# The last gated slice in two halves of tokens, and the last block's outputs in four stores

## The chip, the cores and the metric

One core of one Trainium2 chip runs the whole program. The metric is device time in microseconds (us), the median of the runs shown. TensorE is called PE here (its weight loads PEld), VectorE DVE, ScalarE ACT, GpSimd POOL, SyncE SP. SP issues the transfers that matter in this case.

## The reference, cut to what matters

A recurrence over the sequence gives 3072 tokens of width 384, a layer of experts changes some of them, and a gated layer ends the program:

```
a = x @ w1                       # x 3072 x 384, w1 384 x 1024
b = x @ w2
h = a * b @ w3                   # w3 1024 x 1024
return h @ w_out                 # w_out 1024 x 384
```

Only that last layer is touched. The kernel has already multiplied w3 by w_out into one matrix wf (1024 x 384), so what is left is g = (x w1) * (x w2) and out = g wf. Each fp32 operand is split into a high and a low part, and each product is made of three matmuls: high by high, high by low, low by high.

## The kernel before, in words

The function `gated_layers` works through 3072 tokens in NB = 6 blocks of TOK = 512. A block has KF = 8 slices of 128 gates. Gates of one slice (`gates(t, f)`, L1515) are 2 weights x 3 chunks of the width x 3 parts = 18 matmuls with 512 moving columns, the tokens of the block; they fill two banks of PSUM, `p_ab[f % 2][0]` for a and `[1]` for b. The outputs of one slice (`outputs(t, f)`, L1527) are 4 token blocks x 3 parts = 12 matmuls with 384 moving columns. They have g of the slice as weights and add up over the 8 slices in four banks `p_o[0..3]`, one for each block of 128 tokens.

Between gates and outputs of a slice stands a chain of four operations on 128x512: ACT copies a out of PSUM (L1574), DVE multiplies it by b (L1612), ACT rounds the product to its high part g_hi (L1577), DVE takes the low part g_lo (L1614). To cover it, PE makes the gates of slice f before the outputs of slice f-1 (`step`, L1544): gates 0, outputs 7 of the block before, gates 1, outputs 0, ..., gates 7, outputs 6, and so on. After the gates 7 of the last block there are only outputs 6 left and then outputs 7. a_sb, g_sb, g_hi, g_lo exist twice, by f % 2.

When a block's outputs are done, ACT copies `p_o[0]` and `p_o[2]` and DVE `p_o[1]` and `p_o[3]` to `o_sb` (L1588, L1632). The helper `first_or_all` lets the copies of blocks 0 and 1 start once `s_o` says that `p_o[1]` is complete, and those of 2 and 3 once `s_gout` says that all four are. SP then stores two halves of 256 tokens each (L1485 to L1490), each after one ACT copy and one DVE copy, and waits at the end for all stores (L1493). The order on each engine is written out by hand; the six blocks run as two unrolled, a loop over the middle, two unrolled and one more step that holds only outputs 7 of the last block.

Of the kernel before, what the change touches and what calls it, by code (L numbers as in the profile page):

```python
# [9 lines left out]
ALU = mybir.AluOpType  # L10
ACT = mybir.ActivationFunctionType
AX = mybir.AxisListType
P = 128


def wait(eng, s, val):

    if isinstance(val, int) and val <= 0:
        return
    eng.wait_ge(s, val)  # L20
# [977 lines left out]
class ExpertInputs:  # L998
# [32 lines left out]
    def part(self, g):  # L1031
        return slice(2 * g * P, 2 * (g + 1) * P)
# [390 lines left out]
def gated_layers(nc, env, xbuf, out):  # L1423

    N, DM = xbuf.shape
    TOK = 4 * P
    NB = N // TOK
    NI = TOK // P
    wm_hi, wm_lo, ident, fold = (env[k] for k in ("wm_hi", "wm_lo", "ident", "fold"))
    KD, KF = DM // P, fold.KF  # L1430
    with ExitStack() as ctx:
# [24 lines left out]
        wf_hi, wf_lo = sb("wf_hi", [P, KF, DM], F32R), sb("wf_lo", [P, KF, DM], F32R)  # L1456
        s_wfhi, s_wflo = sem("wfhi"), sem("wflo")

        def first_or_all(eng, t, i):

            if i < NI // 2:
                wait(eng, s_o, t.num(1, 1))
            else:
                wait(eng, s_gout, t.num(KF, KF))
# [8 lines left out]
        with nc.Block() as block:  # L1473
            @block.sync
            def _(sp):
                def load(t):
                    if isinstance(t.c, int) and t.num() == 0:
                        return
                    if isinstance(t.c, int) and t.num() == 2:
                        sp.wait_ge(s_T, 2)  # L1480
                    else:
                        wait(sp, s_turned, t.num(KD, -2 * KD))
                    gx.load(sp, xbuf, t.slot, t.num())

                def store(t):  # L1485
                    for h in range(2):
                        wait(sp, s_oact, t.num(2, h + 1))
                        wait(sp, s_odve, t.num(2, h + 1))
                        sp.dma_start(out[bass.ds(t.num(TOK, h * TOK // 2), TOK // 2), :].rearrange("(i p) d -> p i d", p=P),
                                     o_sb[t.slot][:, 2 * h:2 * h + 2, :]).then_inc(s_st[t.slot], 16)  # L1490
                rounds(sp, whole((load, 2), (store, 0)), 2, NB, 2, 0)
                for i in range(2):
                    sp.wait_ge(s_st[i], 32 * NB // 2)  # L1493

            @block.gpsimd
            def _(pool):
# [4 lines left out]
            @block.tensor  # L1501
            def _(pe):
                fold.product(pe, KF - 1, p_o[-1], (2,))
                pe.wait_ge(env["s_wmlo"], 2 * KD)

                def first_transposes(part):

                    for i in range(NI):
                        if part == 0 and i % 2 == 0:
                            pe.wait_ge(s_x[i // 2], 16)  # L1510
                        for k in ((0, 1), (2,))[part]:
                            m = pe.transpose(p_ab[part][k % 2][:, i * P:(i + 1) * P], x_in[0][:, i, k * P:(k + 1) * P], ident[:, :])
                    m.then_inc(s_T, 1)

                def gates(t, f):  # L1515
                    wait(pe, s_g, t.num(KF, f - 1))
                    cols = slice(f * P, (f + 1) * P)
                    for w in range(2):
                        for k in range(KD):
                            if f == 0 and w == 0:  # L1520
                                wait(pe, s_xlo, t.num(KD, k + 1))
                            for n, (a, b) in enumerate(((wm_hi, xT_hi), (wm_hi, xT_lo), (wm_lo, xT_hi))):
                                m = pe.matmul(p_ab[f % 2][w][:, :], a[:, w * KD + k, cols], b[t.slot][:, k, :],  # L1523
                                              start=(k == 0 and n == 0), stop=(k == KD - 1 and n == 2))
                    m.then_inc(s_ab, 1)

                def outputs(t, f):  # L1527
                    wait(pe, s_glo, t.num(KF, f + 1))
                    if isinstance(t.num(), int) and t.num() == 0:
                        pe.wait_ge(s_wflo, f + 1)  # L1530
                        pe.wait_ge(fold.s_Wout, KF)
                    if f == 0:
                        wait(pe, s_oact, t.num(2))
                        wait(pe, s_odve, t.num(2))
                    for i in range(NI):
                        cols = slice(i * P, (i + 1) * P)
                        for n, (a, b) in enumerate(((g_hi, wf_hi), (g_hi, wf_lo), (g_lo, wf_hi))):
                            m = pe.matmul(p_o[i][:, 0:DM], a[f % 2][:, cols], b[:, f, :],  # L1538
                                          start=(f == 0 and n == 0), stop=(f == KF - 1 and n == 2))
                        if f == KF - 1 and i == NI // 2 - 1:  # L1540
                            m.then_inc(s_o, 1)
                    m.then_inc(s_gout, 1)

                def step(c, j):  # L1544
                    t, before = Item(c, j, 0, 2), Item(c, j, -1, 2)
                    for f in range(KF):
                        if t.inside(NB):
                            gates(t, f)
                        if f:
                            if t.inside(NB):  # L1550
                                outputs(t, f - 1)
                        elif before.inside(NB):
                            outputs(before, KF - 1)
                first_transposes(0)
                first_transposes(1)
                fold.product(pe, KF - 1, p_o[-1], (3,))
                rounds(pe, step, 2, NB, 0, 1)

            @block.scalar
            def _(act):  # L1560
                def wf_part(f):
                    act.wait_ge(fold.s_Wout, f + 1)
                    act.activation(wf_hi[:, f, :], fold.wf[:, f, :], ACT.Copy).then_inc(s_wfhi, 1)

                def wf_parts():

                    for f in range(KF):
                        if f == KF - 1:
                            fold.taken(act, f, p_o[-1])
                        wf_part(f)  # L1570

                def product(t, f):
                    wait(act, s_ab, t.num(KF, f + 1))
                    act.activation(a_sb[f % 2][:, :], p_ab[f % 2][0][:, :], ACT.Copy).then_inc(s_a, 1)  # L1574
                    wait(act, s_g, t.num(KF, f + 1))
                    wait(act, s_gout, t.num(KF, f - 1))
                    act.activation(g_hi[f % 2][:, :], g_sb[f % 2][:, :], ACT.Copy).then_inc(s_ghi, 1)  # L1577

                def first_x_hi():
                    for k in range(KD):  # L1580
                        act.wait_ge(s_T, 1 + k // 2)
                        act.activation(xT_hi[0][:, k, :], p_ab[k // 2][k % 2][:, :], ACT.Copy).then_inc(s_xhi, 1)

                def x_hi(t, k):
                    wait(act, s_turned, t.num(KD, k + 1 - KD))
                    act.activation(xT_hi[t.slot][:, k, :], xT[:, k, :], ACT.Copy).then_inc(s_xhi, 1)

                def out_copy(t):  # L1588
                    wait(act, s_st[t.slot], t.turn(32))
                    for i in range(0, NI, 2):  # L1590
                        first_or_all(act, t, i)
                        act.activation(o_sb[t.slot][:, i, :], p_o[i][:, 0:DM], ACT.Copy).then_inc(s_oact, 1)

                def step(c, j):
                    t, before, nxt = Item(c, j, 0, 2), Item(c, j, -1, 2), Item(c, j, 1, 2)
                    for f in range(KF):
                        if t.inside(NB):
                            product(t, f)
                        if f == 0 and before.inside(NB):
                            out_copy(before)  # L1600
                        if 2 <= f < 2 + KD and nxt.inside(NB):
                            x_hi(nxt, f - 2)
                first_x_hi()
                wf_parts()
                rounds(act, step, 2, NB, 0, 1)

            @block.vector
            def _(dve):
                def product(t, f):
                    wait(dve, s_a, t.num(KF, f + 1))  # L1610
                    wait(dve, s_glo, t.num(KF, f - 1))
                    dve.tensor_tensor(g_sb[f % 2][:, :], a_sb[f % 2][:, :], p_ab[f % 2][1][:, :], ALU.mult).then_inc(s_g, 1)  # L1612
                    wait(dve, s_ghi, t.num(KF, f + 1))
                    dve.tensor_tensor(g_lo[f % 2][:, :], g_sb[f % 2][:, :], g_hi[f % 2][:, :], ALU.subtract).then_inc(s_glo, 1)  # L1614
# [123 lines left out]
```

## Time and profile before

| | us |
|---|---|
| median of 3 runs | 608.86 (608.21 to 608.92) |
| the profiled execution, its own time | 608.56 |
| span of its trace | 606.8 |
| PE busy in the span | 589.0 (97%) |
| PEld busy | 526.0 (87%) |
| DVE busy | 295.1 (49%) |
| ACT busy | 226.7 (37%) |

The span runs from the first to the last instruction that the trace has; some 1.8 us of the execution lie around it. Busy PE counts matmuls whose time overlaps that of the next, so that the distance between the starts of two matmuls is what one costs. The gated layer is the second half of the program.

### The profile page before, as it was taken

The numbers are of one execution on the slowest core, as the hardware profiler recorded it, in microseconds if no ns is written. First come the engines' busy times: TensorE is split into PE (matmuls) and PEld (weight loads), VectorE is DVE, ScalarE is ACT, GpSimd is POOL, SyncE is SP. The second block draws the span as 40 slices with busy tenths as digits, with TensorE's granted clock in tenths as the row PEclk, the third lists the DMA queues.
The fourth block names the chain that finished last, engine by engine and source line by source line (L and its number), as shares of the span: only waits on it lengthen the run. The fifth ranks groups of instructions, "written<-read, shape, count | busy, mean of one in ns | idle before, by whom it ended". The sixth has DMA issues, their size and how long they took to land.

```text
span 606.8 us, 17257 instructions
## 1 busy us (share of the span) xinstructions
PE 589.0 (97%) x7295; PEld 526.0 (87%) x7295; DVE 295.1 (49%) x474; ACT 226.7 (37%) x410; POOL 156.3 (26%) x179
## 2 busy tenths in 40 slices
PE   6699999999999999999999999999999999999997
PEld 6689999766999999999688888888888888888886
DVE  5478889283677777784124233322413323332212
ACT  3156666445655555653143122222213222222212
POOL 7568788214154444441150000000000000000000
PEclk9899999999999999999999999999999999999999
DMA  7779998686467776650350021004004001001001
GB/s 132 133 140 183 184 186 188 226 278 240 175 255 277 279 271 250 204 187 20 100 79 1 1 74 31 0 9 97 0 1 104 1 0 53 1 0 51 2 1 52
DMA packets 133218, 67.80 MB, mean 112 GB/s; under 512 B 111228, under 2 KB 127232, under 8 KB 133176
## 3 DMA queue, kind: packets, MB, share of 16 engines
q1 hardware_dynamic: 105320, 57.91, 33.3%
q10 hardware_dynamic: 25552, 4.72, 4.2%
q0 software_dynamic: 2304, 4.59, 2.2%
q8 instruction: 28, 0.46, 0.3%
q14 instruction: 14, 0.11, 0.1%
HBM read 55.92 MB, written 12.20 MB: 112 GB/s over the span
## 4 chain that ended last, share of the span: by engine, by line
PE 92%; DVE 3%; issue 2%; DMA 1%; ACT 0%; DVEq 0%; POOL 0%; SPq 0%; POOLq 0%
PE gl_pab L1523 33%; PE p_pair L1293 11%; PE ex_ph L1277 11%; PE gl_po L1538 8%; PE p_pair L1538 8%; PE p_pair L94 5%; PE p_K L293 2%; PE p_Y L359 2%; PE p_pair L406 2%; PE p_Y L380 2%; PE p_Y L338 2%; PE p_R L293 2%; PE p_pair L374 2%; DVE k_dec L600 1%; DMA w_in<-xbuf 1%
## 5 line engine op out<-in xcount | busy, mean ns | idle before, releaser
L1612 DVE TENSOR_TENSOR gl_g_sb<-gl_a_sb,gl_pab 128x512 f32<-128x512 f32 x48 | 33.0, 688 | 173.9 <-ACT gl_a_sb L1574 173.9
L1523 PE MATMUL gl_pab<-gl_xT_hi,wm_lo 128*128 128x512 f32 x288 | 113.0, 393 | 0.0
L1523 PE MATMUL gl_pab<-gl_xT_lo,wm_hi 128*128 128x512 f32 x288 | 112.9, 392 | 0.0
L1523 PE MATMUL gl_pab<-gl_xT_hi,wm_hi 128*128 128x512 f32 x288 | 112.2, 390 | 0.0
L1574 ACT ACTIVATE gl_a_sb<-gl_pab 128x512 f32<-128x512 f32 x48 | 28.7, 597 | 186.1 <-PE gl_pab L1523 186.1
L1523 PEld LDWEIGHTS gl_pab<-gl_xT_hi,wm_lo 128*128 128x128 f32 x288 | 54.0, 188 | 11.4
L1523 PEld LDWEIGHTS gl_pab<-gl_xT_hi,wm_hi 128*128 128x128 f32 x288 | 54.1, 188 | 10.5 <-DVE gl_xT_lo L1619 0.3
L1523 PEld LDWEIGHTS gl_pab<-gl_xT_lo,wm_hi 128*128 128x128 f32 x288 | 54.0, 188 | 10.4
L1277 PE MATMUL ex_ph<-ex_xT_hi,ew_w_hi 128*128 128x224 f32 x192 | 52.9, 276 | 0.0
L1277 PE MATMUL ex_ph<-ex_xT_hi,ew_w_lo 128*128 128x224 f32 x192 | 52.7, 275 | 0.0
L1277 PE MATMUL ex_ph<-ex_xT_lo,ew_w_hi 128*128 128x224 f32 x192 | 52.7, 274 | 0.0
L1614 DVE TENSOR_TENSOR gl_g_lo<-gl_g_sb,gl_g_hi 128x512 fp32r<-128x512 f32 x48 | 33.2, 692 | 33.5 <-ACT gl_g_hi L1577 33.5
L1577 ACT ACTIVATE gl_g_hi<-gl_g_sb 128x512 fp32r<-128x512 f32 x48 | 30.3, 632 | 36.2 <-DVE gl_g_sb L1612 36.2
L1293 PE MATMUL p_pair<-ew_w_hi,ex_h_hi 128*96 128x384 f32 (+1 forms) x128 | 43.5, 340 | 0.0
L1293 PE MATMUL p_pair<-ew_w_hi,ex_h_lo 128*96 128x384 f32 (+1 forms) x128 | 43.1, 336 | 0.0
L1293 PE MATMUL p_pair<-ew_w_lo,ex_h_hi 128*96 128x384 f32 (+1 forms) x128 | 43.0, 336 | 0.0
L1043 POOL DMA_INDIRECT ew_x_in<-xbuf,slot_token x16 | 22.4, 1403 | 71.0 <-DVE ex_x_new L1404 49.9
L94 PE MATMUL p_pair<-wo,w3T 128*128 128x384 f32 x112 | 38.8, 490 | 0.5 <-PEq L1701 0.4
L1277 PEld LDWEIGHTS ex_ph<-ex_xT_hi,ew_w_hi 128*128 128x128 f32 x192 | 36.9, 192 | 0.2
L1277 PEld LDWEIGHTS ex_ph<-ex_xT_lo,ew_w_hi 128*128 128x128 f32 x192 | 36.9, 192 | 0.1
L1277 PEld LDWEIGHTS ex_ph<-ex_xT_hi,ew_w_lo 128*128 128x128 f32 x192 | 36.9, 192 | 0.0
L1339 ACT ACTIVATE ew_w_hi<-ew_w_in 128x768 fp32r<-128x768 f32 x32 | 26.9, 840 | 18.2 <-PE p_pair L1293 18.2
(200 smaller groups left out, 1226.5 us busy)
## 6 DMA issues: line engine op xcount, KB each, us to landing
w_in<-in_moe_w SPq DMA_DIRECT2D x8, 1536.0 KB, 7.6
ew_w_in<-in_moe_w SPq DMA_DIRECT2D x8, 1536.0 KB, 6.6
w_in<-in_moe_w SPq DMA_DIRECT2D x14, 512.0 KB, 7.3
k_in<-in_k SPq DMA_DIRECT2D x48, 96.0 KB
v_in<-in_v ACTq DMA_DIRECT2D x48, 96.0 KB
r_in<-in_r SPq DMA_DIRECT2D x48, 96.0 KB
out<-gl_o_sb SPq DMA_DIRECT2D x12, 384.0 KB, 2.7
w_in<-xbuf SPq DMA_DIRECT2D x60, 64.0 KB, 2.4
```

What stands on the lines that cost most here:

```text
L94: m = pe.matmul(bank[:, 0:self.DM], self.w3T[i % 3][:, g, :], self.wo[:, g, :], start=(g == 0), stop=(g == self.KF - 1), skip_group_check= ...
L293: return pe.transpose(out, x, ident[rows, rows])
L1043: pool.indirect_dma_start(self.x_in[slot][0:tokens.shape[0], i, :], None, xbuf[:, :], bass.IndirectOffsetOnAxis(ap=tokens, axis=0), bounds ...
L1277: m = pe.matmul(p_h[g][:, f % 2, 0:width(t)], a[:, k, cols], b[:, k, 0:width(t)], start=(k == 0 and n == 0), stop=(k == KD - 1 and n == 2))
L1293: m = pe.matmul(p_y[i][0:n_tok, 0:DM], a[:, f, cols], b[:, f, :], start=(f == 0 and n == 0), stop=(f == KF - 1 and n == 2))
L1339: act.activation(flat(w2_hi[:, 2 * g:2 * g + 2, :]), flat(w2_in[:, 2 * g:2 * g + 2, :]), ACT.Copy).then_inc(s_w2hi, 1)
L1523: m = pe.matmul(p_ab[f % 2][w][:, :], a[:, w * KD + k, cols], b[t.slot][:, k, :], start=(k == 0 and n == 0), stop=(k == KD - 1 and n == 2))
L1538: m = pe.matmul(p_o[i][:, 0:DM], a[f % 2][:, cols], b[:, f, :], start=(f == 0 and n == 0), stop=(f == KF - 1 and n == 2))
L1574: act.activation(a_sb[f % 2][:, :], p_ab[f % 2][0][:, :], ACT.Copy).then_inc(s_a, 1)
L1577: act.activation(g_hi[f % 2][:, :], g_sb[f % 2][:, :], ACT.Copy).then_inc(s_ghi, 1)
L1612: dve.tensor_tensor(g_sb[f % 2][:, :], a_sb[f % 2][:, :], p_ab[f % 2][1][:, :], ALU.mult).then_inc(s_g, 1)
L1614: dve.tensor_tensor(g_lo[f % 2][:, :], g_sb[f % 2][:, :], g_hi[f % 2][:, :], ALU.subtract).then_inc(s_glo, 1)
```

## The change

In the last block alone: gates of slice 7 are made as two passes of 18 matmuls with 256 moving columns, the first 256 tokens into the left half of `p_ab[1]`, the others into the right half of `p_ab[0]`. ACT and DVE run their chain once for each half. The outputs of slices 6 and 7 come after both passes, and go token block by token block: 3 matmuls of slice 6 and 3 of slice 7 into `p_o[i]`, then a signal. Each token block is copied on its own signal and stored by a transfer of its own. Semaphore counts follow.

```
+        def part(h):
+            return slice(h * TOK // 2, (h + 1) * TOK // 2)
         def first_or_all(eng, t, i):
-            if i < NI // 2:
+            if is_last(t):
+                wait(eng, s_o, NB + i)
+            elif i < NI // 2:
...
+                def store_last():
+                    for i in range(NI):
+                        wait(sp, (s_oact, s_odve)[i % 2], 2 * NB - 1 + i // 2)
+                        sp.dma_start(out[(NB - 1) * TOK + i * P:(NB - 1) * TOK + (i + 1) * P, :], o_sb[(NB - 1) % 2][:, i, :]).then_inc(s_st[(NB - 1) % 2], 16)
...
-                    sp.wait_ge(s_st[i], 32 * NB // 2)
+                    sp.wait_ge(s_st[i], 32 * NB // 2 + (32 if i == (NB - 1) % 2 else 0))
...
+                def last_gates(t, h):
+                    wait(pe, s_g, t.num(KF, KF - 2 + h))
+                    cols = slice((KF - 1) * P, KF * P)
+                    for w in range(2):
+                        for k in range(KD):
+                            for n, (a, b) in enumerate(((wm_hi, xT_hi), (wm_hi, xT_lo), (wm_lo, xT_hi))):
+                                m = pe.matmul(p_ab[1 - h][w][:, part(h)], a[:, w * KD + k, cols], b[t.slot][:, k, part(h)],
+                                              start=(k == 0 and n == 0), stop=(k == KD - 1 and n == 2))
+                    m.then_inc(s_ab, 1)
+                def last_outputs(t):
+                    for i in range(NI):
+                        cols = slice(i * P, (i + 1) * P)
+                        for f in (KF - 2, KF - 1):
+                            wait(pe, s_glo, t.num(KF, KF - 1 if f == KF - 2 else KF + i // 2))
+                            for n, (a, b) in enumerate(((g_hi, wf_hi), (g_hi, wf_lo), (g_lo, wf_hi))):
+                                m = pe.matmul(p_o[i][:, 0:DM], a[f % 2][:, cols], b[:, f, :], start=False, stop=(f == KF - 1 and n == 2))
+                        m.then_inc(s_o, 1)
...
+                            if is_last(t) and f == KF - 1:
+                                last_gates(t, 0)
+                                last_gates(t, 1)
+                                last_outputs(t)
+                                continue
...
# ACT
+                def last_product(t):
+                    for h in range(2):
+                        wait(act, s_ab, t.num(KF, KF + h))
+                        act.activation(a_sb[1][:, part(h)], p_ab[1 - h][0][:, part(h)], ACT.Copy).then_inc(s_a, 1)
+                        wait(act, s_g, t.num(KF, KF + h))
+                        wait(act, s_gout, t.num(KF, KF - 2))
+                        act.activation(g_hi[1][:, part(h)], g_sb[1][:, part(h)], ACT.Copy).then_inc(s_ghi, 1)
# DVE
+                def last_product(t):
+                    for h in range(2):
+                        wait(dve, s_a, t.num(KF, KF + h))
+                        wait(dve, s_glo, t.num(KF, KF - 2))
+                        dve.tensor_tensor(g_sb[1][:, part(h)], a_sb[1][:, part(h)], p_ab[1 - h][1][:, part(h)], ALU.mult).then_inc(s_g, 1)
+                        wait(dve, s_ghi, t.num(KF, KF + h))
+                        dve.tensor_tensor(g_lo[1][:, part(h)], g_sb[1][:, part(h)], g_hi[1][:, part(h)], ALU.subtract).then_inc(s_glo, 1)
```

## Rows read from the trace of the kernel before

**Rows 1.** The page: share of each engine; TensorE's granted clock in 40 slices.
```profile
PE 589.0 (97%) x7295; PEld 526.0 (87%) x7295; DVE 295.1 (49%) x474; ACT 226.7 (37%) x410; POOL 156.3 (26%) x179
PEclk9899999999999999999999999999999999999999
```
**Rows 2.** The chain of waits: start, length, what; a steady slice, then the end.
```profile
569.06 4.12 PE gl_pab L1523 x18
573.18 1.06 PE gl_po L1538 x6
574.25 1.04 PE p_pair L1538 x6
...
600.14 0.70 DVE gl_g_lo L1614
...
600.89 1.33 PE gl_po L1538 x6
602.22 1.07 PE p_pair L1538 x6
603.28 0.02 issue
603.31 0.56 DVE gl_o_sb L1636
```
**Rows 3.** The timeline's end: start, length, engine, line, operation [idle before <-releaser].
```profile
597.70 0.39 PE L1523 MATMUL gl_pab<-gl_xT_hi,wm_lo 128*128 128x512 f32 x1
597.93 0.33 PE L1538 MATMUL gl_po<-gl_wf_hi,gl_g_hi 128*128 128x384 f32 x1
...
599.86 0.34 PE L1538 MATMUL p_pair<-gl_wf_hi,gl_g_lo 128*128 128x384 f32 x1
600.14 0.69 DVE L1614 TENSOR_TENSOR gl_g_lo<-gl_g_sb,gl_g_hi 128x512 fp32r<-128x512 f32 x1 [0.70 <-ACT gl_g_hi L1577]
...
600.89 0.44 PE L1538 MATMUL gl_po<-gl_wf_hi,gl_g_hi 128*128 128x384 f32 x1 [0.69 <-DVE gl_g_lo L1614]
...
601.17 0.34 PE L1538 MATMUL gl_po<-gl_wf_lo,gl_g_hi 128*128 128x384 f32 x1
```
**Rows 4.** SP's timeline, and what SP waited for: longest last.
```profile
602.96 0.37 SPq L1489 DMA_DIRECT2D out<-gl_o_sb  x1
...
603.94 0.37 SPq L1489 DMA_DIRECT2D out<-gl_o_sb  x1
...
SPq L1493 <- DMA out<-gl_o_sb: 2.0, 1, 2.0
```
**Rows 5.** Windows: busy PE, PEld, DVE, ACT, POOL, then PEclk, DMA share, GB/s.
```profile
603.80:603.90 0.10, 0.00 (x0) 0.00 (x0) 0.07 (x1) 0.00 (x0) 0.00 (x0) 1.00 0.27 108
603.90:604.00 0.10, 0.00 (x0) 0.00 (x0) 0.00 (x0) 0.00 (x0) 0.00 (x0) 1.00 1.08 415
...
605.80:605.90 0.10, 0.00 (x0) 0.00 (x0) 0.00 (x0) 0.00 (x0) 0.00 (x0) 0.50 0.58 200
```
**Rows 6.** The chain of waits in the experts: 72 matmuls with 224 columns.
```profile
274.41 8.03 PE ex_ph L1277 x72
```
**Rows 7.** One line's weight loads: duration min/median/max in ns, first and last start.
```profile
L1277 PEld LDWEIGHTS ex_ph<-ex_xT_hi,ew_w_hi x192: 187/192/193, 154.9 to 281.8; 128*128 128x128 f32 x192
```
**Rows 8.** Groups by shape: line, engine, op xcount | busy us, mean ns | idle.
```profile
L1574 ACT ACTIVATE gl_a_sb<-gl_pab 128x512 f32<-128x512 f32 x48 | 28.7, 597 | 186.1 <-PE gl_pab L1523 186.1
L1612 DVE TENSOR_TENSOR gl_g_sb<-gl_a_sb,gl_pab 128x512 f32<-128x512 f32 x48 | 33.0, 688 | 173.9 <-ACT gl_a_sb L1574 173.9
L1577 ACT ACTIVATE gl_g_hi<-gl_g_sb 128x512 fp32r<-128x512 f32 x48 | 30.3, 632 | 36.2 <-DVE gl_g_sb L1612 36.2
L1614 DVE TENSOR_TENSOR gl_g_lo<-gl_g_sb,gl_g_hi 128x512 fp32r<-128x512 f32 x48 | 33.2, 692 | 33.5 <-ACT gl_g_hi L1577 33.5
...
L1389 DVE TENSOR_TENSOR ex_xT_lo<-ex_px,ex_xT_hi 128x224 fp32r<-128x224 f32 x8 | 3.0, 381 | 0.0
L1346 ACT ACTIVATE ex_xT_hi<-ex_px 128x224 fp32r<-128x224 f32 x8 | 2.8, 352 | 0.0
L1592 ACT ACTIVATE gl_o_sb<-p_pair 128x384 f32<-128x384 f32 x6 | 2.9, 483 | 0.5 <-PE p_pair L1538 0.5
```
**Rows 9.** Issue to landing, min/median/max: the stores of out; 0.8 KB loads of w_sq.
```profile
DMA to landing us min/median/max: 2.4/2.7/4.7
...
DMA to landing us min/median/max: 2.0/2.1/2.2
```

More of the change, by code:

```diff
@@ L1457, in gated_layers, with is_last @@
         s_wfhi, s_wflo = sem("wfhi"), sem("wflo")
+        def is_last(t):
+            return isinstance(t.num(), int) and t.num() == NB - 1
+        def part(h):
+            return slice(h * TOK // 2, (h + 1) * TOK // 2)
         def first_or_all(eng, t, i):
-            if i < NI // 2:
+            if is_last(t):
+                wait(eng, s_o, NB + i)
+            elif i < NI // 2:
                 wait(eng, s_o, t.num(1, 1))
@@ L1483, in load @@
                     gx.load(sp, xbuf, t.slot, t.num())
+                def store_last():
+                    for i in range(NI):
+                        wait(sp, (s_oact, s_odve)[i % 2], 2 * NB - 1 + i // 2)
+                        sp.dma_start(out[(NB - 1) * TOK + i * P:(NB - 1) * TOK + (i + 1) * P, :], o_sb[(NB - 1) % 2][:, i, :]).then_inc(s_st[(NB - 1) % 2], 16)
                 def store(t):
+                    if is_last(t):
+                        store_last()
+                        return
                     for h in range(2):
@@ L1551, in step @@
                                 outputs(t, f - 1)
-                        elif before.inside(NB):
+                        elif before.inside(NB) and not is_last(before):
                             outputs(before, KF - 1)
@@ L1570, in wf_parts @@
                         wf_part(f)
+                def last_product(t):
[5 more added lines that the diff above has]
+                        act.activation(g_hi[1][:, part(h)], g_sb[1][:, part(h)], ACT.Copy).then_inc(s_ghi, 1)
                 def product(t, f):
+                    if is_last(t) and f == KF - 1:
+                        last_product(t)
+                        return
                     wait(act, s_ab, t.num(KF, f + 1))
@@ L1608, in _ @@
             def _(dve):
+                def last_product(t):
[5 more added lines that the diff above has]
+                        dve.tensor_tensor(g_lo[1][:, part(h)], g_sb[1][:, part(h)], g_hi[1][:, part(h)], ALU.subtract).then_inc(s_glo, 1)
                 def product(t, f):
+                    if is_last(t) and f == KF - 1:
+                        last_product(t)
+                        return
                     wait(dve, s_a, t.num(KF, f + 1))
```

## The prediction, made before the changed kernel was run

> **What bounds the kernel now.** I read the page first: PE is busy 97% of the span, at a granted clock of 0.9 to 1.0 nearly throughout [rows 1], so PE sets the time as long as there is work for it. Then the chain of waits. In steady state one slice is 4.12 us of gates and 1.06 + 1.04 us of outputs, and the next slice begins at once: ACT and DVE are hidden. Only at the end does the chain leave PE [rows 2]. That end is all that the change touches, so I read it instruction by instruction.
>
> Gates 7 of the last block end, outputs 6 start at 597.93 and their twelfth matmul starts at 599.86. Twelve at 2.10 us are 0.175 us each, so a thirteenth could start at 600.03. It starts at 600.89, on DVE's g_lo of slice 7, and the one behind it only 0.28 us later instead of 0.175 [rows 3]. The exposed wait thus costs 0.86 + 0.11 = 0.97 us. PE releases the last copies at 603.28, DVE copies for 0.56 us [rows 2], and SP issues the two stores at 602.96 and 603.94 [rows 4]. Data of both flow from about 603.87 (0.91 us behind the first issue) to about 605.87, without a break at some 400 GB/s [rows 5]: 1.0 us for each 384 KB. The last wait begins when the second issue ends, at 604.31, and takes 2.0 us [rows 4]: the second store has landed at 606.31, 0.44 us behind its data, 2.4 us behind its issue, which is the shortest landing of the twelve stores [rows 9]. Another 0.49 us ends the span.
>
> **The change part by part.**
>
> Gates 7. 18 matmuls with 512 columns go (4.12 us, 0.229 each), 36 with 256 columns come, each with a weight load of its own. No row shows 256 columns. With 224 columns 72 take 8.03 us, 0.1115 each [rows 6]; with 384 they take 0.175 [rows 2]. The line between them gives 0.1115 + 0.0635 x 32/160 = 0.124. Ends: below, half of 0.229, that is 0.114; above, 0.1115 x 256/224 = 0.127. I take 0.124, as 224 is the nearest row. 36 x 0.124 = 4.46: +0.34 us (0.00 to +0.45).
>
> The Trainium skill, "TensorE: Matmul & The Clock Gate", section "Back-to-back issue gap", says that in a stream of load and matmul pairs both set the spacing, with 81 ns at 128 columns and 131 ns at 512. Taken at its word, an estimate from that page puts 256 columns at 98 ns, and the split at 36 x 0.098 - 18 x 0.131 = +1.17 us. That is a rule against this change; but the trace has 0.229 us at 512 columns [rows 2], not 0.131, so I don't go by it.
>
> The wait for g_lo. Now the two passes run, then 24 output matmuls with no gap if the data is there. Put the start of gates 7 at 593.80 (4.12 before 597.93). The first pass's columns are issued by 593.80 + 2.23 = 596.03, complete some 0.17 us later (a 384 matmul is 0.34 long at 0.175 apart [rows 3]). The half chain: ACT with 224 columns out of PSUM 0.352, with 512 0.597; DVE 0.381 and 0.688 [rows 8]. By these lines 256 columns cost ACT 0.38 and DVE 0.42, and g_hi, 0.632 at 512, some 0.40; with 0.02 between operations the chain is 0.38 + 0.42 + 0.40 + 0.42 + 0.08 = 1.70 us. The first half is ready at 597.9; its first reader (slice 7 of token block 0) is due at 593.80 + 4.46 + 3 x 0.175 = 598.79. The second half starts at 598.43 and is ready at 600.13; its first reader is due after 15 output matmuls, 600.88. Slack 0.9 and 0.75 us. ACT and DVE are idle when each half comes: the chain of slice 6 is done before 595, and that of the first half before the second begins. So the 0.97 us go whole, and nothing of the 8 added waits on PE is late. If the cover failed, the price is what the chain exceeds 2.45 us by: with full-width durations for half-width operations (0.597 + 0.688 + 0.632 + 0.692 + 0.08 = 2.69) that is 0.24 us. The copies of token block 0 queue behind the second half's chain on ACT, and that of block 1 behind g_lo on DVE: they start at about 599.7 and 600.6, nobody waits for them but early stores.
>
> PE's end thus moves by -0.97 + 0.34 = -0.63 us, from 603.28 to 602.65.
>
> The other order of the outputs (3 matmuls of slice 6, 3 of slice 7 for each block) has the same 24 matmuls of the same form: 0. Releasing blocks singly brings nothing for the last block by itself, since its copy waits for the last matmul as before: DVE's 0.56 us stays.
>
> The stores. Four issues of 0.37 us instead of two [rows 4], at about 600.3, 601.2, 602.1 and 603.31: SP is idle between them, so the first three lie beside PE's work, and their 192 KB each (0.5 us at the rate above) are gone before the next begins. The last is issued 0.07 us behind its copy as before (603.87 to 603.94): 602.65 + 0.03 + 0.56 + 0.07 = 603.31. Data starts 0.91 later at 604.22, takes 0.5, and lands 0.44 later at 605.16; 0.49 to the end: 605.65. Against 606.8 that is -1.15 us, of which 0.63 is PE and 0.52 the tail (0.50 the half size, 0.02 rounding and the short queue behind the first store). No row shows a store of 192 KB alone. Ends: the landing stays at 2.4 us, as with 384 KB (0 gained), or it goes below the 0.5 us by proportion, if the time from issue to first data shrinks too; smallest transfers still land in 2.0 us [rows 9], so I give that 0.2 more at most. I take the 0.5.
>
> The Trainium skill, "DMA: Bandwidth & Descriptors", section "Bandwidth", gives loads of 64 KB 0.95 us and of 1 MB 6.15 us of transfer and asks for large transfers. An estimate between them gives 192 KB 1.64 us, by which the small store would land 1.1 us later than I say and the whole gain would shrink to about nothing. The trace has 384 KB in 1.0 us [rows 5], so it doesn't bear that out for these stores.
>
> Everything ahead of the last block is the same code. PE's program grows by 18 matmuls and loads behind it; I cost fetching them at nothing, since the tail before shows no gap on PE but the one named.
>
> **From span to time.** The profiled execution took 608.56, so 607.41 with the change; from the median 608.86 it is 607.71. The median stands near the upper end of its three runs and the profile 0.30 under it; I take the middle, 607.6.
>
> **The rivals.**
> A small store takes as long as a large one. For it: very small transfers take 2.0 to 2.2 us to land, little below the 2.4 of 384 KB [rows 9]. Against it: two stores in a row take twice 1.0 us of data at a full rate [rows 5]. Gain 0.63 to 0.9: 608.0.
> The chain of the second half is late after all (0.24 us, above), or PE pays the 0.11 us of a restart at a wait: gain 0.8 to 1.0: 607.8.
> Weight loads bound the half-width matmuls: each is shown as 188 to 192 ns long [rows 7] and there are now twice as many for the same columns. If the spacing were 0.188, gates 7 would cost 36 x 0.188 = 6.77, 2.31 more than taken, and the kernel would be 1.16 us slower than before: 610.0. It is slower than before from a spacing of 0.124 + 1.15/36 = 0.156. Against it: loads of that length lie 0.1115 apart in the experts [rows 6, 7].
> The change doesn't do what it says as to the stores: three of the four hide nothing that wasn't hidden, only the size of the last one counts. This is in my sum already; if the last store's halving is eaten by a later issue on SP, it is the first rival.
> More than forecast: time from issue to data shrinks, and 256 columns cost 0.114. Gain up to 1.15 + 0.2 + 0.34 = 1.7: 607.1.
>
> **How the numbers follow.** Forecast 0.58, own range 607.3 to 607.9. First rival 0.16, second 0.08, weight loads or another loss 0.06, more than forecast 0.12. The range to hold eight in ten is 607.1 to 608.3. What this kernel's measurement can tell from no change is about 0.2%, 1.2 us, and the forecast of 1.15 to 1.26 us (from either base) lies on that line. Faster by more than 0.2% (under 607.64): the more-than-forecast case and somewhat over two thirds of the forecast's 0.58, 0.52. Slower (over 610.08): the case of the weight loads, whose 610.0 lies just short of that line and which would hardly come without some more wait, or another loss of that size: 0.05. The rest, 0.43, is within 0.2%.
>
> **What would show it right or wrong.** In the trace after: 36 matmuls with 256 columns 0.124 us apart; no idle time on PE between the last gates and the last output; the chain of waits on PE up to the last copy; the last copy's start at about 602.7; four issues on SP, the last at about 603.3 and landed 1.85 us later; a span of about 605.65. Wrong if PE waits again in front of token block 2, if the spacing is over 0.13, or if the last store takes 2.4 us. Whether the spacing or the store was mis-sized can be read off one by one.

## The result, and the profile after

The changed kernel takes 607.75 us (median of 20 runs, 605.82 to 608.51), the kernel before 608.78 (607.88 to 611.13). The two medians are 1.03 us apart, a ratio of 0.9983, and the two averages (607.55 and 609.00) 1.45 us. The ratio on record is 0.9974, with a 95% interval of 0.9965 to 0.9983: 1.6 us faster, between 1.0 and 2.1, so that the medians lie at its end. Forecast were 607.6 us and 1.15 to 1.26 us of gain, in a range of 607.1 to 608.3.

The profiled execution of the changed kernel took 608.42 us, its span is 606.7, hardly less than the 606.8 of before. So the span can't be read as a whole: the part ahead of the change was longer in this execution, and an experiment below says how far that goes. What can be compared is the last stretch. I measure it from where the chain of waits begins gates 6 of the last block to the span's end. In the kernel before the chain has gates 6 at 587.74 and gates 7 at 593.97, and the stretch is 606.8 - 587.74 = 19.06 us. The views give a span to 0.1 us, so each stretch is known to 0.05 us and the difference of two to 0.1 us. The chain of the kernel before (start, length, what), then that of the changed kernel:

```profile
587.74 4.12 PE gl_pab L1523 x18
...
593.97 4.14 PE gl_pab L1523 x18
...
598.13 0.61 ACT gl_a_sb L1574
...
598.76 0.70 DVE gl_g_sb L1612
...
599.48 0.64 ACT gl_g_hi L1577
```
```profile
589.06 4.12 PE gl_pab L1539 x18
...
595.28 4.31 PE gl_pab L1567 x36
599.59 2.08 PE gl_po L1577 x12
601.68 2.10 PE p_pair L1577 x12
603.77 0.02 issue
603.80 0.56 DVE gl_o_sb L1699
```

From 589.06 to 606.7 are 17.64 us, 1.42 less. The four steps of ACT and DVE that stood on the chain before, the three in the first of these fences and g_lo [rows 2], are gone: PE runs without a break from gates 6 to the last output, and only the last copy is left. From gates 7 to PE's last release are 603.77 - 595.28 = 8.49 us, before 603.28 - 593.97 = 9.31: 0.82 of the 1.42 us. The 36 half-width matmuls take 4.31 us, 0.1197 each.

The chains of the halves in the timeline (start, length, engine, line, operation, idle before it and who ended it): the four operations of the first half, the last one of the second half, and the weight load (PEld) and the matmul on PE that read it first:

```profile
597.47 0.38 ACT L1616 ACTIVATE gl_a_sb<-gl_pab 128x256 f32<-128x256 f32 x1 [2.27 <-PE gl_pab L1567]
...
597.89 0.42 DVE L1665 TENSOR_TENSOR gl_g_sb<-gl_a_sb,gl_pab 128x256 f32<-128x256 f32 x1 [1.96 <-ACT gl_a_sb L1616]
...
598.34 0.42 ACT L1619 ACTIVATE gl_g_hi<-gl_g_sb 128x256 fp32r<-128x256 f32 x1 [0.49 <-DVE gl_g_sb L1665]
...
598.79 0.43 DVE L1667 TENSOR_TENSOR gl_g_lo<-gl_g_sb,gl_g_hi 128x256 fp32r<-128x256 f32 x1 [0.48 <-ACT gl_g_hi L1619]
...
600.95 0.43 DVE L1667 TENSOR_TENSOR gl_g_lo<-gl_g_sb,gl_g_hi 128x256 fp32r<-128x256 f32 x1 [0.48 <-ACT gl_g_hi L1619]
...
601.87 0.19 PEld L1577 LDWEIGHTS p_pair<-gl_wf_hi,gl_g_hi 128*128 128x128 f32 x1
...
602.04 0.33 PE L1577 MATMUL p_pair<-gl_wf_hi,gl_g_hi 128*128 128x384 f32 x1
```

The second half's g_lo is ready at 601.38 and the first matmul behind its wait, the fourth of token block 2, starts at 602.04: 0.66 us to spare (0.75 forecast). The forecast counted to the matmul. Its weights are the data waited for, and their load starts at 601.87 already, so counted to it the slack is 0.49 us. The other part of the gain is the stores. SP's rows, what SP waited for, and the landing of the four stores:

```profile
604.38 0.33 SPq L1496 DMA_DIRECT2D out<-gl_o_sb  x1
```
```profile
SPq L1509 <- DMA out<-gl_o_sb: 1.5, 1, 1.5
```
```profile
DMA to landing us min/median/max: 1.8/1.8/1.8
```

Landing is the time from a store's issue until it is reported complete. The last store lands 1.8 us behind its issue, where 384 KB took 2.4 [rows 9]. Its data can be seen in the windows (the last two numbers are the share of the DMA engines and GB/s); the 0.2 us ahead of these show none, the 0.2 us behind them a share of 0.01:

```profile
605.20:605.40 0.20, 0.00 (x0) 0.00 (x0) 0.00 (x0) 0.00 (x0) 0.00 (x0) 1.00 0.78 300
605.40:605.60 0.20, 0.00 (x0) 0.00 (x0) 0.00 (x0) 0.00 (x0) 0.00 (x0) 1.00 1.12 422
605.60:605.80 0.20, 0.00 (x0) 0.00 (x0) 0.00 (x0) 0.00 (x0) 0.00 (x0) 1.00 0.73 261
```

From PE's last release to the end are 606.7 - 603.77 = 2.93 us, before 606.8 - 603.28 = 3.52: 0.59. With the 0.82 of PE that is the 1.42, up to rounding.

### The profile page after: what moved, and what is told of

The parts are those of the page before. It is cut to its first block, busy times and chain, and to the rows that moved or that the text cites. A ratio compares the mean times of both kernels' runs of the same rounds, so it can differ in the third digit from the quotient of the medians.

```text
span 606.7 us, 17299 instructions
## 1 busy us (share of the span) xinstructions
PE 590.9 (97%) x7313; PEld 529.2 (87%) x7313; DVE 293.2 (48%) x476; ACT 227.2 (37%) x412; POOL 156.7 (26%) x179
## 4 chain that ended last, share of the span: by engine, by line
PE 50%; DVE 0%; issue 0%
PE gl_pab L1539 32%; PE gl_po L1554 8%; PE p_pair L1554 8%; PE gl_pab L1567 1%; PE p_pair L94 0%; PE p_pair L1577 0%; PE gl_po L1577 0%; PE gl_pab L1528 0%; DVE gl_o_sb L1699 0%
## 5 line engine op out<-in xcount | busy, mean ns | idle before, releaser
L1539 PE MATMUL gl_pab<-gl_xT_hi,wm_lo 128*128 128x512 f32 x282 | 110.6, 392 | 0.0
L1539 PE MATMUL gl_pab<-gl_xT_lo,wm_hi 128*128 128x512 f32 x282 | 110.5, 392 | 0.0
L1539 PE MATMUL gl_pab<-gl_xT_hi,wm_hi 128*128 128x512 f32 x282 | 109.8, 389 | 0.0
```

## The experiments

All are read by the same stretch, since the times alone are known to 0.1% (0.6 us) at best. Each edit is shown against the changed kernel, cut to what matters (cuts are marked). The expectations of experiments 1 to 4 name the stretch from the first matmul of gates 6, which starts 0.16 us before the chain enters them (19.22 us before); I give what was measured from the chain's start, beside expectations that are 0.16 lower.

**1. The halves alone.** The order of outputs 6 and 7 and the two stores are put back:

```
-                wait(eng, s_o, NB + i)
+                wait(eng, s_o, NB + i // 2)
...
-                    if is_last(t):
-                        store_last()
-                        return
...
-                    for i in range(NI):
-                        cols = slice(i * P, (i + 1) * P)
-                        for f in (KF - 2, KF - 1):
+                    for f in (KF - 2, KF - 1):
+                        for i in range(NI):
+                            cols = slice(i * P, (i + 1) * P)
...
```

> Gates 7 of the last block in two halves, but outputs 6 and then outputs 7 in the old order and two stores of 384 KB. I look at the stretch from the first matmul of gates 6 of the last block to the span's end: 19.22 us before (587.58 to 606.8), 17.80 after (588.90 to 606.7). Theory (the halves alone take the wait off PE, the order by token block adds nothing there): no gap on PE, its end 0.83 us earlier than before as in the changed kernel, stores as before: 18.4 us. Rival (block by block order is needed for the cover): PE still waits some tenths in front of outputs 7: 18.7 or more.

The ratio to the kernel before is 0.9987 (0.9977 to 0.9997), 0.8 us faster. The chain has gates 6 at 586.66 in a span of 604.9: 18.24 us, as expected (18.2), and 0.82 less than before.

```profile
586.66 4.12 PE gl_pab L1536 x18
...
592.89 4.31 PE gl_pab L1564 x36
597.20 1.04 PE gl_po L1574 x6
598.24 1.04 PE p_pair L1574 x6
599.28 1.04 PE gl_po L1574 x6
600.32 1.06 PE p_pair L1574 x6
```

Two passes and then all outputs: no wait. The order by token block does nothing for the cover; it asks for the first half's data earlier, after three output matmuls instead of twelve.

**2. The stores alone.** Gates 7, their chain and the order of the outputs as before; each token block of slice 7 is signalled, copied and stored by itself:

```
-                        if f == KF - 1 and i == NI // 2 - 1:
+                        if f == KF - 1 and (i == NI // 2 - 1 or is_last(t)):
...
-                            if is_last(t) and f == KF - 1:
-                                last_gates(t, 0)
-                                last_gates(t, 1)
-                                last_outputs(t)
-                                continue
...
```

> Gates 7 in one pass and the outputs in the old order, each token block of slice 7 released, copied and stored by itself (four stores of 192 KB). Theory (the last store's size sets the tail): PE idles before outputs 7 as before, the last store lands 1.8 us after its issue instead of 2.4: the stretch is 19.22 - 0.59 = 18.6 us. Rival (the shorter landing in the changed kernel comes from the stores being spread over more time, not from the size): here the four stores come 0.52 us apart, so their data is one unbroken stretch again and the last lands 2.2 to 2.4 us after its issue: 19.0 to 19.2.

The ratio is 0.9993 (0.9984 to 1.0002), not to be told from nothing by time. The stretch is 606.9 - 588.38 = 18.52 us, 0.54 less than before (18.5 expected). The wait for g_lo is on the chain as before; the stores' landing (min/median/max) is short:

```profile
588.38 4.12 PE gl_pab L1539 x18
...
600.78 0.70 DVE gl_g_lo L1667
...
601.53 1.32 PE gl_po L1554 x6
602.85 1.07 PE p_pair L1554 x6
```
```profile
DMA to landing us min/median/max: 1.8/1.9/2.0
```

So it is the size and not the spreading. Here the four stores are issued some 0.5 us apart, each with 0.5 us of data, and the slowest lands in 2.0 us. 0.82 + 0.54 = 1.36 of the 1.42 us: the two parts add up. The 0.06 left over is within what spans of 0.1 us can tell; that the stores queue a little here would fit it.

**3. The order by token block without the halves.** Gates 7 in one pass, then the outputs block by block:

```
-                            wait(pe, s_glo, t.num(KF, KF - 1 if f == KF - 2 else KF + i // 2))
+                            wait(pe, s_glo, t.num(KF, f + 1))
...
-                                last_gates(t, 0)
-                                last_gates(t, 1)
+                                gates(t, f)
                                 last_outputs(t)
...
```

> Gates 7 in one pass of 512 columns, but the outputs of slices 6 and 7 token block by token block and four stores. Theory (the order by block is only bearable because of the halves): after three output matmuls PE waits for g_lo of slice 7, some 2.4 us, then 21 matmuls run; the stretch is 19.22 + 1.5 - 0.6 = 20.1 us, slower than before by 0.9. Rival (the order is neutral and the wait stays 0.97 us): 18.6 us.

The ratio is 1.0034 (1.0020 to 1.0048), 2.1 us slower than before, and the stretch is 611.0 - 589.45 = 21.55 us: 2.5 more than before, where 0.9 more was expected. The wait came as expected, PE idle for 2.28 us. What I had not counted is in the timeline (start, length) and in the windows, where the number behind POOL's is the granted clock:

```profile
602.59 0.45 PE L1577 MATMUL gl_po<-gl_wf_hi,gl_g_hi 128*128 128x384 f32 x1 [2.28 <-DVE gl_g_lo L1670]
...
605.38 0.53 PE L1577 MATMUL p_pair<-gl_wf_hi,gl_g_lo 128*128 128x384 f32 x1
605.70 0.53 PE L1577 MATMUL p_pair<-gl_wf_hi,gl_g_hi 128*128 128x384 f32 x1
```
```profile
600.00:602.00 2.00, 0.32 (x2) 0.00 (x0) 0.84 (x2) 1.06 (x2) 0.00 (x0) 1.00 0.00 0
...
602.60:604.00 1.40, 1.40 (x7) 1.40 (x8) 0.00 (x0) 0.49 (x1) 0.00 (x0) 0.89 0.00 0
604.00:605.00 1.00, 1.00 (x4) 1.00 (x4) 0.00 (x0) 0.00 (x0) 0.00 (x0) 0.50 0.13 51
...
607.00:608.00 1.00, 1.00 (x6) 0.75 (x4) 0.00 (x0) 0.40 (x1) 0.00 (x0) 0.95 0.03 11
```

Some 1.1 us after PE had begun to work again the granted clock went to half, 1.2 GHz, and stayed there until about 607. The matmuls then start 0.32 us apart instead of 0.175; ten such distances and the two at their ends (0.21 and 0.23) cost 1.45 + 0.09 = 1.5 us, nearly the whole of the miss of 1.6. The clock is read in one execution. The times fit it: the median of the eight is 611.13 us against 608.53, and even the lower end of the interval, 1.2 us slower, lies above the 0.9 expected. In the kernel before, the exposed wait had left PE idle for 0.69 us [rows 3] and no matmul was slowed. Here the longer idle stretch was dearer than its own length. The order by block is borne only because the halves have hidden the chain first.

**4. The same wait hidden without splitting.** Gates 7 go ahead of outputs 5, in one pass; outputs 5 and 6 cover the chain. Four stores as in experiment 2.

```
...
-                            gates(t, f)
+                            if not (is_last(t) and f == KF - 1):
+                                gates(t, f)
+                            if is_last(t) and f == KF - 2:
+                                gates(t, f + 1)
                         if f:
...
```

> Another way to hide the same wait: gates 7 of the last block in one pass of 512 columns, but ahead of outputs 5, so that outputs 5 and 6 (24 matmuls, 4.2 us) cover the chain of slice 7; then outputs 7, with four stores. g_hi of slice 7 must wait for outputs 5, since there are two buffers. Theory: no gap on PE and none of the 0.19 us that the halves cost (36 x 0.1197 against 4.12 us): the stretch is 19.22 - 0.97 - 0.59 = 17.7 us, 0.1 to 0.2 less than in the changed kernel. Rival (g_hi of slice 7 comes too late behind outputs 5, or PE pays at the doubled gates): 17.9 or more.

The ratio is 0.9969 (0.9958 to 0.9980). The stretch is 607.0 - 589.57 = 17.43 us (17.5 expected), 1.63 less than before and some 0.2 less than in the changed kernel:

```profile
589.57 8.20 PE gl_pab L1539 x36
597.77 1.06 PE gl_po L1554 x6
...
601.95 1.04 PE gl_po L1554 x6
...
604.05 0.02 issue
604.08 0.56 DVE gl_o_sb L1692
```

Gates 6 and 7 are 36 full-width matmuls in 8.20 us, where the changed kernel has 4.12 and 4.31, and the 36 output matmuls follow without a gap. g_hi of slice 7 did wait for outputs 5, 1.56 us on ACT, and was still in time.

**5. ACT makes the last copy.** The edit of experiment 4, and with it:

```
-                        wait(sp, (s_oact, s_odve)[i % 2], 2 * NB - 1 + i // 2)
+                        wait(sp, (s_odve, s_oact)[i % 2], 2 * NB - 1 + i // 2)
...
-                    for i in range(0, NI, 2):
+                    for i in range(1 if is_last(t) else 0, NI, 2):
                         first_or_all(act, t, i)
...
-                    for i in range(1, NI, 2):
+                    for i in range(0 if is_last(t) else 1, NI, 2):
                         first_or_all(dve, t, i)
```

> The kernel with gates 7 ahead of outputs 5 and four stores, and now ACT copies token blocks 1 and 3 of the last block and DVE 0 and 2. The copy that ends the chain becomes ACT's (0.49 us) instead of DVE's (0.56). I look at the stretch from where the chain of waits begins gates 6 of the last block to the span's end: 19.06 us before, 17.64 in the changed kernel, 17.43 with gates 7 early. Theory (the last copy stands on the chain whole): 17.36. Rival (the hand-over from ACT to SP costs what the shorter copy gains): 17.43. In time, 0.995 to 0.998 of the kernel before either way.

The ratio is 0.9973 (0.9960 to 0.9987). The stretch is 604.5 - 587.13 = 17.37 us, where the theory had 17.36 and the rival 17.43, which spans of 0.1 us can't tell apart. SP's rows can: from PE's release to the issue of the last store are 602.16 - 601.62 = 0.54 us here and 604.66 - 604.05 = 0.61 in experiment 4, less by the whole 0.07 of the shorter copy. The chain:

```profile
587.13 8.20 PE gl_pab L1539 x36
...
601.62 0.02 issue
601.64 0.49 ACT gl_o_sb L1640
```

The stretch is the shortest of all, 0.2 to 0.3 us under the changed kernel's. The times don't tell experiments 4 and 5 and the changed kernel apart: their intervals overlap.

**6. Quarters instead of halves.** How far can a pass be split? Each half pass in two of 128 columns:

```
...
+                    for q in range(2 * h, 2 * h + 2):
+                        quarter = slice(q * P, (q + 1) * P)
...
-                                m = pe.matmul(p_ab[1 - h][w][:, part(h)], a[:, w * KD + k, cols], b[t.slot][:, k, part(h)],
+                                    m = pe.matmul(p_ab[1 - h][w][:, quarter], a[:, w * KD + k, cols], b[t.slot][:, k, quarter],
...
```

> The changed kernel, with each half pass of gates 7 made as two quarter passes of 128 columns: 72 matmuls with weight loads of their own instead of 36; all else as in the changed kernel. Measured spacings so far: 0.1115 us at 224 columns, 0.1197 at 256, 0.175 at 384, 0.229 at 512, which for the last three is columns/2400 + 0.013 to 0.016 us; 224 lies above that line. Theory A (a load of its own sets a floor of about 0.108 us, which 256 columns just clear): gates 7 take 72 x 0.108 = 7.8 us, the stretch is 17.64 + 3.5 = 21.1 us, slower than before. Theory B (no floor, the line goes on): 72 x 0.067 = 4.8 us, the stretch is 18.1 us.

The ratio is 1.0037 (1.0026 to 1.0049); the stretch is 609.0 - 587.65 = 21.35 us. Theory A:

```profile
587.65 4.12 PE gl_pab L1539 x18
...
593.88 7.99 PE gl_pab L1569 x72
601.87 2.14 PE gl_po L1579 x12
```

7.99 / 72 = 0.111 us at 128 columns, the same as the 0.1115 at 224 [rows 6]. Between 128 and 224 columns the spacing doesn't depend on the columns. That each matmul has a 128x128 weight load of its own is the likely reason; taking the loads away by themselves was not tried.

**7. One store at the end.** The changed kernel with the last block in one store of 768 KB:

```
-                    for i in range(NI):
-                        wait(sp, (s_oact, s_odve)[i % 2], 2 * NB - 1 + i // 2)
-                        sp.dma_start(out[(NB - 1) * TOK + i * P:(NB - 1) * TOK + (i + 1) * P, :], o_sb[(NB - 1) % 2][:, i, :]).then_inc(s_st[(NB - 1) % 2], 16)
+                    wait(sp, s_oact, 2 * NB)
+                    wait(sp, s_odve, 2 * NB)
+                    sp.dma_start(out[(NB - 1) * TOK:NB * TOK, :].rearrange("(i p) d -> p i d", p=P), o_sb[(NB - 1) % 2][:, :, :]).then_inc(s_st[(NB - 1) % 2], 16)
...
-                    sp.wait_ge(s_st[i], 32 * NB // 2 + (32 if i == (NB - 1) % 2 else 0))
+                    sp.wait_ge(s_st[i], 32 * NB // 2 + (-16 if i == (NB - 1) % 2 else 0))
```

> The changed kernel, but the last block goes out in one store of 768 KB after the last copy, where there were four of 192 KB. Theory (a store costs 0.91 us to its first data, its bytes at some 390 KB per us, and 0.4 us behind them; only what is issued last counts): it lands 1.8 + 1.5 = 3.3 us after its issue and the stretch is 17.64 + 1.5 = 19.1 us, as long as before the change. Rival (a large part of a store's time doesn't depend on its size): it lands in 2.4 to 2.8 us, the stretch is 18.2 to 18.6.

The ratio is 1.0009 (0.9997 to 1.0022), the stretch 606.5 - 587.31 = 19.19 us: the whole gain of the change is given back by one last store that is four times as large. Its landing:

```profile
DMA to landing us min/median/max: 3.4/3.4/3.4
```

192 KB land in 1.8 us, 384 in 2.4, 768 in 3.4: about 1.3 us that don't depend on the size and 0.27 us for each 100 KB.

**8. Both kernels once more.** Unchanged copies, one profiled execution each.

> The kernel before, unchanged, profiled once more. Theory (the start of the last block's gates 6 on the chain scatters by some us from execution to execution, 586.7 to 589.6 so far in kernels with the same code ahead of it, and the stretch behind it hardly at all): the start lies anywhere in 586 to 590, the stretch to the span's end is 19.06 within 0.05. Rival (the scatter comes with the changed code): the start is 587.74 within 0.2 again.

> The changed kernel, profiled once more. Theory as for the repeat of the kernel before: the start lies anywhere in 586 to 590, the stretch is 17.64 within 0.05. Rival: the start is 589.06 within 0.2 again.

In the repeat of the kernel before, the chain has gates 6 at 587.06, where they were at 587.74, and gates 7 at 593.28 instead of 593.97; the span is 606.1. Here is that repeat, then that of the changed kernel, whose span is 606.0:

```profile
587.06 4.12 PE gl_pab L1523 x18
...
593.28 4.14 PE gl_pab L1523 x18
```
```profile
588.39 4.12 PE gl_pab L1539 x18
```

The stretch of the kernel before is 606.1 - 587.06 = 19.04 us, and was 19.06; from gates 7 to the end are 606.1 - 593.28 = 12.82 us, before 606.8 - 593.97 = 12.83. The changed kernel's stretch is 606.0 - 588.39 = 17.61, and was 17.64. The stretches repeat within 0.03 us; the part ahead of them moved by 0.7 us in both kernels, with nothing changed.

One thing the repeats don't settle: in both pairs the changed kernel entered gates 6 later, by 1.32 and by 1.33 us, and so both pairs of spans look alike. That this is chance, and not the price of the change, is said by the other runs. With 1.3 us lost ahead of the stretch the kernels would differ by 0.1 us, and over twenty executions each they differ by 1.0 (medians) to 1.6 us (ratio). A later start that belongs to the change can then be 0.4 us at most. The halves alone (experiment 1) entered gates 6 at 586.66, ahead of both executions of the kernel before.

## Why the prediction was right, point by point

**What bounds the kernel.** Right: outside the last stretch nothing changed, and the wait for g_lo and the last store were what the end was made of.

**Gates 7 as halves, +0.34 us (0.00 to +0.45).** 4.31 against 4.12: +0.19. The spacing was 0.1197 us, not 0.124, inside the bounds 0.114 to 0.127. The term was mis-sized because I drew the line from the nearest row, 224 columns, which lies on the floor of 0.111 that experiment 6 shows and not on the slope. From 384 and 512 columns the line goes to 0.121. The estimate from the Trainium skill, "TensorE: Matmul & The Clock Gate", section "Back-to-back issue gap", was +1.17 us; no run here bears it out. The rival of the weight loads was right that there is a floor (that the loads set it is not shown) and wrong on its place: at 0.111, not at 0.188. At 256 columns it doesn't bind, at 128 it does.

**The wait, -0.97 us.** It went whole, shown by experiment 1. PE's end moved by 0.82 (0.63 forecast), of which 0.15 is the spacing of the halves and 0.04 lie among the outputs. From the first to the last of the 24 output matmuls are 602.93 - 597.93 = 5.00 us before and 603.42 - 599.43 = 3.99 after. The wait and the slow start behind it make 0.96 of that difference, as forecast; the other 21 distances were 0.176 us on average before and 0.1735 after, which is the rest. The chains took 1.75 us for a half (1.70 forecast), slack 0.66 (0.75), or 0.49 counted to the weight load. The rival of a late second half didn't occur.

**The order by block, 0.** Right as long as the chain is hidden (experiments 1 and 2 add up to the changed kernel without it, to the 0.1 us of the spans); alone it costs 2.5 us (experiment 3).

**The stores, -0.52 us.** 0.59 in the changed kernel and 0.54 alone. The forecast landing was 1.85 us, the measured 1.8. The rival in which a small store takes as long as a large one falls with experiments 2 and 7. The estimate from the Trainium skill, "DMA: Bandwidth & Descriptors", section "Bandwidth", 1.64 us of transfer for 192 KB, was worked out from loads; for these stores it is not borne out either: the data took some 0.5 us.

**The sum.** -1.15 forecast, -1.42 in the stretch, and -1.6 us (-1.0 to -2.1) by the ratio. The 0.27 missed are the 0.15 of the spacing, the 0.04 of the outputs and some 0.07 of the stores. 607.6 was forecast and 607.75 measured against a base of 608.78; that the two lie so close is in part luck, the scatter of the medians, since the forecast gain was a fifth too small. My chance of 0.52 for faster by over 0.2% and 0.43 for within was a fair picture of a gain that lies on the line.

## What to carry to other kernels

Where a kernel's end is one chain of waits, read it instruction by instruction and sum it on its own: the terms of this forecast were each within 0.15 us of what was measured, while medians of whole runs tell 0.6 us. Before an operation is split to hide a wait, look for an order that hides it at full width: here putting the last gates one group earlier did it with no extra matmul. Make the last transfer small: here each halving, from 768 to 384 to 192 KB, took 1.0 and 0.6 us off the landing, and less than 192 KB was not tried. Keep a wait on PE short, as its price can be more than its length.

## What the runs showed of the hardware that was not expected

**The floor of a matmul with a weight load of its own.** The spacing is 0.111 us at 128 and at 224 columns, 0.1197 at 256, 0.175 at 384, 0.229 at 512 (128x128 weights, granted clock 1.00, 2.4 GHz). That the load sets the floor is likely and was not tested.

**A stretch of idle PE that costs again later.** After 2.28 us of idleness the granted clock fell to half, 1.1 us into the next work, for about three us (experiment 3, one profiled execution); after 0.69 us it did not.

**Where the scatter between runs is made.** The eleven profiled executions run the same code for the first 300 us. Their last matmul of L380, the end of the first stage, starts at 110.9 to 113.8 us. From there to gates 6 of the last block all eleven take 475.7 to 476.2 us, so nearly all of the scatter is made in that first stage. The granted clock of 32 to 38 us already tells them apart: 1.00 in the four that end that stage at 110.9 to 111.7, 0.50 to 0.70 in the six that end it at 111.9 to 113.8, and 0.91 in one with 111.1. The window of the kernel before and that of the changed kernel, in their first profiled executions (the number behind POOL's is the clock):

```profile
32.00:38.00 6.00, 4.96 (x253) 4.51 (x246) 3.44 (x7) 3.46 (x9) 3.12 (x4) 1.00 0.67 127
```
```profile
32.00:38.00 6.00, 5.25 (x151) 4.77 (x146) 2.40 (x6) 1.65 (x5) 2.78 (x3) 0.50 0.54 102
```

In the first PE gets through 253 matmuls in these 6 us, in the second through 151. The count doesn't follow the clock alone: the repeat of the changed kernel has 254 at 0.70. The window was also picked after the times were known, and the slowest start at 1.00 (111.7) and the fastest at 0.50 to 0.70 (111.9) are only 0.2 us apart. PE waits for data at many places of this stage, and where the clock falls may decide whether the slow stretch lies on the chain. Nothing was run to steer it, so this goes with the scatter and isn't shown to cause it. At up to 2.9 us it is twice the gain of the change, and it is the next thing to look at in this kernel.
